# A mixture-of-experts stage whose tiles hold one or two blocks of 128 places

## The chip, the cores and the metric

The kernel runs on one core of a Trainium2 chip. A core has TensorE (PE in the profile; PEld is its weight load), VectorE (DVE), ScalarE (ACT), GpSimd (POOL) and SyncE (SP), which run side by side, keep time by semaphores and share 16 DMA engines. The metric is the device time of one execution in microseconds; less is better.

## The reference

Three computations follow one another: a recurrent attention over 4 x 768 tokens, a mixture of experts with two experts for each token, and a dense network of two layers. The change lies in the second.

```python
def _moe_ref(x, w_gate, w_noise, noise, w1, w2):
    N, D = x.shape            # 3072 tokens, 320 wide; 8 experts, 1024 wide inside
    ...
    top2 = np.argpartition(-noisy_logits, 2, axis=1)[:, :2]
    ...
    for e in range(E):
        for k in range(2):
            mask = top2[:, k] == e
            ...
            h = np.maximum(x[mask] @ w1[e], 0.0)
            out[mask] += top2_w[mask, k, None] * (h @ w2[e])
    return out
```

## The kernel before

The program has three stages, one behind the other. `stage_a` is the attention and leaves each token's row in `xrow` and the gate logits in `LG`. `stage_re` chooses two experts for each token, gives each of the 6144 choices a place in a list ordered by expert, and runs the experts over that list, tile by tile. `stage_m` gathers each token's two results from `ysort`, adds them with their gate weights and runs the dense network.

**Placing.** The list is cut in tiles of `TS` = 256 places, and each expert begins at a new tile. `NTS` = 31 tiles are enough for any choice, and all 31 are always run, whatever the experts' counts are. VectorE counts the choices of each expert (`run`, `cnt`), turns the counts into tiles (`ntile`, `endt`), and from these into each choice's place (`base`, `off`, `pf`, `pos`, L1166 to L1187) and each tile's expert (`ge`, `tef`, `texp`). For the inverse, which token stands in a place, it builds comparisons of the place's low seven bits (`lows`, L1202, four instructions) and of its block of 128 (`highs`, L1194 and L1196 in `columns`, first six blocks and then the rest), and TensorE multiplies them (L1016, 48 matmuls for the six blocks, 48 for the rest). ScalarE copies the first six blocks' tokens to `src` (L1035), VectorE the rest (L1212). GpSimd gathers the tokens' rows to `xs` by them (L1088), SyncE loads the expert's weights by `texp` (L931, L933 the first, L950 the second).

**One tile.** Weights and rows are float32; each is split into a high part of type float32r (ScalarE, `split_hi`, L830) and the rest (VectorE, `split_lo`, L835), and a product takes three matmuls, high by high, high by low and low by high. TensorE runs, for each of `NF` = 8 groups `f` of 128 inner columns, the first layer's eight matmuls (L986 to L990, 256 columns each) into one of four banks; then the six transposes of the next tile's rows (`turn`, L970); then the second layer, for each `f` and each of two blocks `s` three matmuls of 320 columns (L1001 to L1003) into the banks 6 and 7. Beside the first layer ScalarE and VectorE split the second weights (`w2h`, `w2l`) and apply the ReLU and split its result (`hh` L1045, `hl` L1120), in turn for each `f`. Behind the transposes they split the next rows (`xh`, `xl`) and the next first weights (`w1h`, `w1l`), and every second tile a slice of the dense network's weights (`wih`, `woh`, `wil`, `wol`). The split weights have one buffer, so the next first weights are split only after the first layer, and the second weights only after the second; unsplit first weights (`w1t`) and rows (`xs`) have two buffers, unsplit second weights (`w2t`) one, which SyncE loads when VectorE has split the last of the tile before. ScalarE and VectorE carry the result to `ys` (L1058, L1136), and SyncE stores it in `ysort` (L937).

The order of all this is written out by hand. The first two tiles and the last stand alone, the others run in loops (`tiles`), two tiles in each turn, since the buffers alternate. `link` on VectorE makes an instruction wait for the one before.

Of the kernel before, what the change touches and what calls it, by code (L numbers as in the profile page):

```python
# [34 lines left out]
E = 8  # L35
# [6 lines left out]
NTS = (2 * TOK + E * (TS - 1)) // TS  # L42
# [795 lines left out]
def stage_re(nc, st, w_in, w_out, w1, w2, xrow, ysort):  # L838
    ctx = ExitStack()
    with ctx:  # L840
# [11 lines left out]
        NSL, NHI = NT * 128 // TS, NTS * TS // 128  # L852
        NH0 = 6

# [39 lines left out]
        iexp, prev, cnt, ntile, endt, base = (small(E) for _ in range(6))  # L894
        isl, gt = small(NSL), small(E, NSL)
        idx, posl, posh = small(NT, 8).bitcast(U32), small(2, NT).bitcast(U32), small(2, NT).bitcast(U32)
# [6 lines left out]
        ge, tef = small(NTS, E)[0:1], small(NTS)[0:1]  # L903

        ld = [sem("e_ld0"), sem("e_ld1")]
        gx = [sem("e_gx0"), sem("e_gx1")]
        wr = [sem("e_wr0"), sem("e_wr1")]
# [4 lines left out]
        yv = ysort.rearrange("(n s p) m -> n p s m", p=128, s=NS)  # L912
        w2v = w2.rearrange("e (f p) m -> e p f m", p=128)
        LD, GX = 3 * 16, NS * 16

        def tiles(eng, tile):
            tile(0, 0, 0, True, False)
            tile(1, 1, 0, True, False)
            with eng.Fori(1, NTS // 2) as n:
                tile(n * 2, 0, n, False, False)  # L920
                tile(n * 2 + 1, 1, n, False, False)
            tile(NTS - 1, 0, NTS // 2, False, True)

        @block.sync
        def _(sp):
            def tile(i, p, n, first, final):
# [7 lines left out]
                if not first:  # L934
                    sp.wait_ge(q["e_yA"], i - 1)
                    sp.wait_ge(q["e_yV"], i - 1)
                    sp.dma_start(yv[bass.ds(i - 2, 1)].rearrange("o p s m -> (o p) s m"), ys[:, p, :, :]).then_inc(wr[p], 16)  # L937
# [16 lines left out]
            for i in (NTS - 2, NTS - 1):  # L954
                sp.wait_ge(q["e_yA"], i + 1)
                sp.wait_ge(q["e_yV"], i + 1)
                sp.dma_start(yv[i], ys[:, i % 2, :, :]).then_inc(wr[i % 2], 16)
# [4 lines left out]
        def _(pe):  # L962
            mm = nc.tensor.matmul

            def turn(i, p, n):
                pe.wait_ge(gx[p], n * GX + GX)
# [6 lines left out]
            def tile(i, p, n, first, final):  # L973
                if first and p == 0:
                    turn(0, 0, 0)
                pe.wait_ge(q["e_xl"], i * 2 + 2)
                pe.wait_ge(q["e_w1l"], i * 3 + 3)
                for f in range(NF):
                    fs = slice(f * 128, f * 128 + 128)
                    o = ps[2 + f % 4][:, 0:TS]  # L980
# [4 lines left out]
                    for j in range(2):  # L985
                        mm(o, w1h[:, j, fs], xh[:, j, :], start=(j == 0), stop=False)  # L986
                        mm(o, w1h[:, j, fs], xl[:, j, :], start=False, stop=False)  # L987
                        mm(o, w1l[:, j, fs], xh[:, j, :], start=False, stop=False)  # L988
                    mm(o, w1h[:, 2, fs], xh[:, 2, :], start=False, stop=False)
                    mm(o, w1l[:, 2, fs], xh[:, 2, :], start=False, stop=True).then_inc(q["e_mm1"], 1)  # L990
                if not final:
                    turn(i + 1, 1 - p, n + p)
# [28 lines left out]
        def _(act):  # L1021
            def rows_and_w1(i, p, n):
                act.wait_ge(q["e_tr"], i + 1)
                split_hi(nc, xh[:, 0:2, :].rearrange("k j s -> k (j s)"), ps[0][:, :]).then_inc(q["e_xh"], 1)
                split_hi(nc, xh[0:64, 2, :], ps[1][0:64, 0:TS]).then_inc(q["e_xh"], 1)
# [3 lines left out]
            def tile(i, p, n, first, final):  # L1029
# [12 lines left out]
                for f in range(NF):  # L1042
                    split_hi(nc, w2h[:, f, :], w2t[:, f, :]).then_inc(q["e_w2h"], 1)
                    act.wait_ge(q["e_mm1"], i * NF + f + 1)
                    nc.scalar.activation(hh[:, f, :], ps[2 + f % 4][:, 0:TS], ACT.Relu).then_inc(q["e_hh"], 1)  # L1045
                if not final:
                    act.wait_ge(ld[1 - p], (n + p) * LD + LD)
                    rows_and_w1(i + 1, 1 - p, n + p)
# [20 lines left out]
        def _(pool):  # L1069
            iota = nc.gpsimd.iota  # L1070
            iota(iexp, pattern=[[1, E]], base=0, channel_multiplier=0, allow_small_or_imprecise_dtypes=True).then_inc(q["r_io"], 1)
            iota(isl, pattern=[[TS, NSL]], base=0, channel_multiplier=0, allow_small_or_imprecise_dtypes=True).then_inc(q["r_io"], 1)
            iota(itl, pattern=[[1, NHI]], base=0, channel_multiplier=0, allow_small_or_imprecise_dtypes=True).then_inc(q["r_io"], 1)
            iota(i128, pattern=[[1, 128]], base=0, channel_multiplier=0, allow_small_or_imprecise_dtypes=True).then_inc(q["r_io"], 1)
            iota(ids, pattern=[[128, NT]], base=0, channel_multiplier=1, allow_small_or_imprecise_dtypes=True).then_inc(q["r_io"], 1)
            pool.wait_ge(q["r_io"], 5)
# [3 lines left out]
            pool.wait_ge(q["r_src0"], 1)  # L1080
            for i in range(NTS):
                if i == NH0 // NS:
# [3 lines left out]
                for s in range(NS):  # L1086
                    t = NS * i + s
                    pool.indirect_dma_start(out=xs[:, i % 2, s, :], out_offset=None, in_=xrow[:, :],  # L1088
                                            in_offset=bass.IndirectOffsetOnAxis(ap=src[:, t:t + 1], axis=0)).then_inc(gx[i % 2], 16)

        @block.vector
        def _(dve):
# [7 lines left out]
            def rows(i, p):  # L1100
                dve.wait_ge(q["e_xh"], i * 2 + 1)
                split_lo(nc, xl[:, :, :].rearrange("k j s -> k (j s)"), ps[0][:, :],
                         xh[:, 0:2, :].rearrange("k j s -> k (j s)")).then_inc(q["e_xl"], 1)
                dve.wait_ge(q["e_xh"], i * 2 + 2)
                split_lo(nc, xh[64:128, 2, :], ps[1][0:64, 0:TS], xh[0:64, 2, :]).then_inc(q["e_xl"], 1)
# [7 lines left out]
            def tile(i, p, n, first, final):  # L1113
                if first and p == 0:
                    rows(0, 0)
                for f in range(NF):
# [3 lines left out]
                    nc.vector.scalar_tensor_tensor(hl[:, f, :], ps[2 + f % 4][:, 0:TS], 0.0, hh[:, f, :].bitcast(F32),  # L1120
# [386 lines left out]
```

## Time and profile before

| | before |
|---|---|
| three runs | 1484.06 us median (1479.6 to 1484.7) |
| profiled execution | 1484.37 us |
| its span | 1482.5 us, mean granted TensorE clock 0.916 |
| PE busy | 1294.8 us (87%) |
| PEld busy | 1177.1 us (79%) |
| DVE, ACT, POOL busy | 936.5, 656.1, 278.1 us |
| DMA | 197.77 MB, mean 133 GB/s |

The span is the time from the first to the last instruction of the profiled execution; the execution's own time is 1.9 us more. A granted clock of 1.00 is 2.4 GHz and 0.50 is 1.2 GHz. Busy times are means over stages that have different limits, so the table doesn't say what bounds a stage.

### The profile page before, as it was taken

The numbers are of one execution on the slowest core, as the hardware profiler recorded it, in microseconds if no ns is written. First come the engines' busy times: TensorE is split into PE (matmuls) and PEld (weight loads), VectorE is DVE, ScalarE is ACT, GpSimd is POOL, SyncE is SP. The second block draws the span as 40 slices with busy tenths as digits, with TensorE's granted clock in tenths as the row PEclk, the third lists the DMA queues.
The fourth block names the chain that finished last, engine by engine and source line by source line (L and its number), as shares of the span: only waits on it lengthen the run. The fifth ranks groups of instructions, "written<-read, shape, count | busy, mean of one in ns | idle before, by whom it ended". The sixth has DMA issues, their size and how long they took to land. (4 is left out here: it accounts for less than half of the span.)

```text
span 1482.5 us, 40880 instructions
## 1 busy us (share of the span) xinstructions
PE 1294.8 (87%) x16814; PEld 1177.1 (79%) x16814; DVE 936.5 (63%) x1619; ACT 656.1 (44%) x1453; POOL 278.1 (19%) x238
## 2 busy tenths in 40 slices
PE   4468788787989873999999999999949999999998
PEld 3357576666767663999999999999938888888987
DVE  8969485784837007577887878878734444455433
ACT  3334343343543222366776766667613332333332
POOL 1015251432522211211111111111033022020000
PEclk9988787887889975799999999999979999999999
DMA  8572535536242302678777787788612011010000
GB/s 232 137 165 92 144 123 127 171 110 155 87 111 86 113 26 66 186 229 266 229 239 255 222 267 221 248 243 234 218 56 60 19 37 52 3 53 18 0 18 18
DMA packets 158556, 197.77 MB, mean 133 GB/s; under 512 B 62581, under 2 KB 117085, under 8 KB 158429
## 3 DMA queue, kind: packets, MB, share of 16 engines
q1 hardware_dynamic: 133492, 147.96, 33.5%
q10 hardware_dynamic: 19657, 29.90, 6.6%
q0 software_dynamic: 5280, 18.03, 4.3%
q8 instruction: 103, 1.69, 0.5%
q14 instruction: 24, 0.20, 0.0%
HBM read 171.53 MB, written 24.31 MB: 132 GB/s over the span
## 5 line engine op out<-in xcount | busy, mean ns | idle before, releaser
L347 DVE TENSOR_TENSOR prod<-Tl,Lt 128x1 f32<-128x1 f32 (+30 forms) x186 | 143.9, 774 | 59.5 <-DMA Lt<-lscr 53.4
L1295 DVE TENSOR_TENSOR gf<-psM,low 128x512 f32<-128x512 f32 x96 | 66.3, 691 | 181.2 <-ACT low L1333 169.5
L1333 ACT ACTIVATE low<-psM 128x512 f32<-128x512 f32 x96 | 57.5, 599 | 244.4 <-PE psM L1391 223.7
L1001 PE MATMUL psE<-w2h,hh 128*128 128x320 f32 x496 | 155.7, 314 | 0.0
L1003 PE MATMUL psE<-w2h,hl 128*128 128x320 f32 x496 | 153.3, 309 | 0.0
L1002 PE MATMUL psE<-w2l,hh 128*128 128x320 f32 x496 | 153.2, 309 | 0.0
L986 PE MATMUL psE<-xh,w1h 128*128 128x256 f32 x496 | 141.3, 285 | 1.9 <-DVE xh L835 1.9
L987 PE MATMUL psE<-xl,w1h 128*128 128x256 f32 x496 | 141.1, 284 | 0.0
L988 PE MATMUL psE<-xh,w1l 128*128 128x256 f32 x496 | 141.0, 284 | 0.0
L1088 POOL DMA_INDIRECT xs<-xrow,src x62 | 60.9, 983 | 409.5 <-PE psE L970 371.0
L835 DVE TENSOR_TENSOR w2l<-w2t,w2h 128x320 fp32r<-128x320 f32 x248 | 121.9, 492 | 17.5 <-ACT w2h L830 17.5
L1370 PE MATMUL psM<-woh,gh 128*128 128x320 f32 x384 | 120.3, 313 | 4.2 <-DVE gl L835 3.6
L1120 DVE SCALAR_TENSOR_TENSOR hl<-psE,hh 128x256 fp32r<-128x256 f32 x248 | 105.1, 424 | 22.6
L1372 PE MATMUL psM<-woh,gl 128*128 128x320 f32 x384 | 118.7, 309 | 0.0
L1371 PE MATMUL psM<-wol,gh 128*128 128x320 f32 x384 | 118.5, 309 | 0.0
L830 ACT ACTIVATE w2h<-w2t 128x320 fp32r<-128x320 f32 x248 | 114.9, 463 | 6.3 <-DMA w2t<-in_w_dram 5.8
L1045 ACT ACTIVATE hh<-psE 128x256 fp32r<-128x256 f32 x248 | 95.2, 384 | 47.3 <-PE psE L990 46.0
L835 DVE TENSOR_TENSOR w1l<-w1t,w1h 128x1024 fp32r<-128x1024 f32 (+1 forms) x93 | 108.1, 1217 | 2.0
L986 PEld LDWEIGHTS psE<-xh,w1h 128*128 128x128 f32 x496 | 95.9, 193 | 2.3 <-DVE xh L835 2.3
L351 DVE TENSOR_REDUCE Tl<-prod 128x1 f32<-128x1 f32 (+30 forms) x186 | 93.7, 504 | 5.9
L830 ACT ACTIVATE w1h<-w1t 128x1024 fp32r<-128x1024 f32 x93 | 91.4, 1050 | 13.4 <-DMA w1t<-in_w_dram 13.4
L988 PEld LDWEIGHTS psE<-xh,w1l 128*128 128x128 f32 x496 | 95.9, 193 | 0.0
(184 smaller groups left out, 3125.3 us busy)
## 6 DMA issues: line engine op xcount, KB each, us to landing
w2t<-in_w_dram SPq DMA_DIRECT2D x31, 1280.0 KB, 6.8
w1t<-in_w_dram SPq DMA_DIRECT2D x31, 1024.0 KB, 8.7
w1t<-in_w_dram SPq DMA_DIRECT2D x62, 256.0 KB, 9.4
Vd<-in_vG_dram ACTq DMA_DIRECT2D x44, 320.0 KB, 5.3
ysort<-ys SPq DMA_DIRECT2D x31, 320.0 KB, 4.9
RV<-in_rvE_dram ACTq DMA_DIRECT2D x44, 208.0 KB
P<-in_wR_dram SPq DMA_DIRECT2D x24, 209.6 KB
U<-in_wE_dram SPq DMA_DIRECT2D x24, 209.6 KB
```

The costliest lines, as they stand in the source:

```text
L347: mark(nc.vector.tensor_tensor(prod[:, 0:t, 0:t], Tl[:, 0:t, CH - t:CH], Lt[:, t:t + 1, CH - t:CH].to_broadcast([128, t, t]), ALU.mult))
L830: return nc.scalar.activation(hi, src, ACT.Copy)
L835: return nc.vector.tensor_tensor(lo, src, hi.bitcast(F32), ALU.subtract)
L986: mm(o, w1h[:, j, fs], xh[:, j, :], start=(j == 0), stop=False)
L987: mm(o, w1h[:, j, fs], xl[:, j, :], start=False, stop=False)
L988: mm(o, w1l[:, j, fs], xh[:, j, :], start=False, stop=False)
L1001: mm(o, hh[:, f, sl], w2h[:, f, :], start=(f == 0), stop=False)
L1002: mm(o, hh[:, f, sl], w2l[:, f, :], start=False, stop=False)
L1003: m = mm(o, hl[:, f, sl], w2h[:, f, :], start=False, stop=(f == NF - 1))
L1370: mm(o, gh[:, f % 4, sl], woh[:, f, :], start=(f == 0), stop=False)
L1371: mm(o, gh[:, f % 4, sl], wol[:, f, :], start=False, stop=False)
L1372: m = mm(o, gl[:, f % 4, sl], woh[:, f, :], start=False, stop=(f == NF - 1))
```

## The change

A tile may now hold two blocks of 128 places (a pair) or one (a single). An expert's choices begin at a new block, not at a new tile of 256. With blocks of 128, 55 blocks (`NBK`) are enough for any choice; they are run as 23 pairs (`NPR`) and 9 singles (`NSG`), so as 32 tiles. An expert's pairs stand from the front of the list, and where it has an odd block, that one is counted from the end (`send`, `sidx`, `delta`).

The order is fixed in the code (`place`): of every four tiles the second is a single, and in the last four the second and the third. The loops take four tiles a turn. A single runs the same loops with 128 columns in the first layer (`W`), one block in the second, three transposes instead of six, and one gather instead of two; its weights are loaded and split as before. VectorE's copy to `ys` is a memset of one element there.

The table of the tiles' experts now comes from `experts()`, which VectorE runs between the first half and the second half of `lows`; before, its instructions stood in the placement arithmetic.

```diff
-NTS = (2 * TOK + E * (TS - 1)) // TS
+NBK = (2 * TOK + E * 127) // 128
+NSG = 9
+NPR = (NBK - NSG) // 2
+NTS = NPR + NSG
...
-        NSL, NHI = NT * 128 // TS, NTS * TS // 128
+        NSL, NHI = NT, NBK + 1
...
+        def place(u, c, tail):
+            if c == 0 or (c > 1 and not tail):
+                return True, u * 3 + (0, 0, 1, 2)[c]
+            if c == 3:
+                return True, NPR - 1
+            return False, u + c - 1
...
-            with eng.Fori(1, NTS // 2) as n:
-                tile(n * 2, 0, n, False, False)
-                tile(n * 2 + 1, 1, n, False, False)
-            tile(NTS - 1, 0, NTS // 2, False, True)
+            with eng.Fori(1, NU - 1) as u:
+                for c in range(4):
+                    tile(u, c, False, False, False)
+            for c in range(4):
+                tile(NU - 1, c, False, c == 3, True)
...
-                    for s in range(NS):
+                    for s in range(NS if pair else 1):
                         c0 = (j % 2) * TS + s * 128
                         m = nc.tensor.transpose(ps[j // 2][0:kr, c0:c0 + 128], xs[:, p, s, k0:k0 + kr], ident[:, :])
...
+                W = TS if pair else 128
...
-                        mm(o, w1h[:, j, fs], xh[:, j, :], start=(j == 0), stop=False)
...
+                        mm(o, w1h[:, j, fs], xh[:, j, 0:W], start=(j == 0), stop=False)
...
                     pe.wait_ge(q["e_w2l"], i * NF + f + 1)
-                    for s in range(NS):
+                    for s in range(NS if pair else 1):
                         o, sl = ps[6 + s][:, 0:DM], slice(s * 128, s * 128 + 128)
...
-                if i == NH0 // NS:
+                pair, at = place(i // 4, i % 4, i // 4 == NU - 1)
+                if i == 3:
                     pool.wait_ge(q["r_src"], 1)
...
-                nc.vector.tensor_copy(ys[:, p, 1, :], ps[7][:, 0:DM]).then_inc(q["e_yV"], 1)
+                if pair:
+                    nc.vector.tensor_copy(ys[:, p, 1, :], ps[7][:, 0:DM]).then_inc(q["e_yV"], 1)
+                else:
+                    nc.vector.memset(ys[0:1, p, 1, 0:1], 0.0).then_inc(q["e_yV"], 1)
...
+            link(tt(run, pf, thr.rearrange("p (e o) -> p e o", o=1).to_broadcast([128, E, NT]), ALU.is_ge))
+            link(tt(run, run, delta.rearrange("p (e o) -> p e o", o=1).to_broadcast([128, E, NT]), ALU.mult))
+            link(tt(pf, pf, run, ALU.add))
...
+            def experts():
...
+                tt(ge, blk[0:1].rearrange(one_row, o=1).to_broadcast([1, NTS, E]),
+                   pend2[0:1].rearrange("p (o e) -> p o e", o=1).to_broadcast([1, NTS, E]), ALU.is_ge)
...
+                link(ts(tef, tef, float(E - 1), None, ALU.min))
+                nc.vector.tensor_copy(texp[:, :], tef).then_inc(q["r_tx"], 1)
+
             for j in range(2):
+                if j:
+                    experts()
                 for f in (slice(0, 12), slice(12, 24)):
                     tt(lows[:, j, f, :], i128.rearrange("p (o t) -> p o t", o=1).to_broadcast([128, 12, 128]),
...
-        ysort = nc.dram_tensor("ysort", [NTS * TS, DM], F32, kind="Internal").ap()
+        ysort = nc.dram_tensor("ysort", [NBK * 128, DM], F32, kind="Internal").ap()
```

Three places show the new order. The first is VectorE in the placement arithmetic, before, from the table comparison to the position:

```order
L1169 SCALAR_TENSOR_TENSOR w2t<-xs,w2t 128x8
L1170 TENSOR_TENSOR xs<-ys,w2t 1x248
L1172 TENSOR_TENSOR ys<-ys 128x192
L1173 TENSOR_TENSOR w2t<-w2t 128x8
L1174 TENSOR_REDUCE xs<-xs 1x31
L1175 SCALAR_TENSOR_TENSOR w2t<-w2t 128x8
L1176 TENSOR_SCALAR xs<-xs 1x31
L1177 TENSOR_TENSOR ys<-ys,w2t 128x192
L1178 CAST texp<-xs 1x31
L1180 TENSOR_TENSOR ys<-psE,ys 128x192
```

and now (here from the scan of the ends; `w2t`, `xs` and `ys` lend their memory to the small arrays):

```order
L1230 SCALAR_TENSOR_TENSOR w2t<-xs,w2t 128x8
L1231 TENSOR_TENSOR w2t<-w2t 128x8
L1232 TENSOR_TENSOR ys<-ys 128x192
L1233 TENSOR_SCALAR w2t<-w2t 128x8
L1234 TENSOR_TENSOR w2t<-w2t 128x8
L1235 SCALAR_TENSOR_TENSOR w2t<-w2t 128x8
L1236 SCALAR_TENSOR_TENSOR w2t<-w2t 128x8
L1237 TENSOR_TENSOR ys<-ys,w2t 128x192
L1239 TENSOR_TENSOR ys<-psE,ys 128x192
L1240 TENSOR_TENSOR ys<-ys,w2t 128x192
L1241 TENSOR_TENSOR ys<-ys,w2t 128x192
L1242 TENSOR_TENSOR ys<-ys 128x192
```

The rows 1 wide (the tile table) are gone from here, and the three of 192 elements behind `psE` and more rows 8 wide have come.

The second is VectorE at the comparisons: `woh` are the `highs`, `wih` the `lows`. Before:

```order
L1194 TENSOR_TENSOR woh<-ys,w2t 128x48x6
L1196 TENSOR_TENSOR woh<-woh,w2t 128x48x6
L1202 TENSOR_TENSOR wih<-w2t 128x1536 x4
L1194 TENSOR_TENSOR woh<-ys,w2t 128x48x56
L1196 TENSOR_TENSOR woh<-woh,w2t 128x48x56
```

and now, from inside `experts()` on:

```order
L1266 TENSOR_TENSOR xs<-w2t 1x256
L1268 TENSOR_TENSOR xs<-w2t 1x256
L1270 TENSOR_REDUCE xs<-xs 1x32
L1271 TENSOR_REDUCE w2t<-xs 1x32
L1272 TENSOR_TENSOR w2t<-w2t,xs 1x32
L1273 TENSOR_SCALAR w2t<-xs 1x32
L1274 TENSOR_TENSOR w2t<-w2t 1x32
L1275 TENSOR_TENSOR xs<-xs,w2t 1x32
L1276 TENSOR_SCALAR xs<-xs 1x32
L1277 CAST texp<-xs 1x32
L1283 TENSOR_TENSOR wih<-w2t 128x1536 x2
L1256 TENSOR_TENSOR woh<-ys,w2t 128x48x50
```

`texp` is now written between the two halves of the `lows` (the other two `wih` stand ahead of `experts()`), and the second `highs` are 50 blocks wide.

The third is TensorE from the first layer's end to the second layer, before:

```order
L990 MATMUL psE5<-xh,w1l 128x256
L970 MATMUL psE0<-ident,xs 128x128 x4
L970 MATMUL psE1<-ident,xs 64x128 x2
L1001 MATMUL psE6<-w2h,hh 128x320
L1002 MATMUL psE6<-w2l,hh 128x320
L1003 MATMUL psE6<-w2h,hl 128x320
L1001 MATMUL psE7<-w2h,hh 128x320
```

and now, in a single that is followed by a pair:

```order
L1031 MATMUL psE5<-xh,w1l 128x128
L1009 MATMUL psE0<-ident,xs 128x128 x4
L1009 MATMUL psE1<-ident,xs 64x128 x2
L1042 MATMUL psE6<-w2h,hh 128x320
L1043 MATMUL psE6<-w2l,hh 128x320
L1044 MATMUL psE6<-w2h,hl 128x320
L1042 MATMUL psE6<-w2h,hh 128x320
```

The first layer's matmuls have 128 columns, and the second layer stays on bank 6, where it went on to bank 7.

## Rows read from the trace of the kernel before

**Rows 1.** Windows of two stages; columns: span, busy us (count) by engine, PEclk, DMA share, GB/s

```profile
563.00:608.85 45.85, 23.82 (x106) 22.76 (x106) 33.68 (x125) 7.50 (x11) 9.71 (x13) 0.50 0.24 64
608.85:1087.00 478.15, 478.13 (x3652) 477.87 (x3652) 377.91 (x724) 321.99 (x708) 54.61 (x57) 1.00 0.75 235
```

**Rows 2.** Waits in the expert stage: total us, times, longest

```profile
ACT w2h L830 <- DMA w2t<-in_w_dram: 5.8, 2, 4.9
```

**Rows 3.** Timeline of PE, one tile; columns: start, us, engine, line, operation, tiles, count

```profile
1056.75 0.28 PE L986 MATMUL psE<-xh,w1h 128*128 128x256 f32 x1
...
1064.42 0.82 PE L970 MATMUL psE<-ident,xs 128*128 128x128 f32 x6
1065.00 0.39 PE L1001 MATMUL psE<-w2h,hh 128*128 128x320 f32 x1
...
1072.12 0.28 PE L986 MATMUL psE<-xh,w1h 128*128 128x256 f32 x1
```

**Rows 4.** Timeline of DVE in the same tile

```profile
1065.91 0.69 DVE L835 TENSOR_TENSOR xl<-psE,xh 128x512 fp32r<-128x512 f32 x1 [0.45 <-ACT xh L830]
...
1067.12 3.49 DVE L835 TENSOR_TENSOR w1l<-w1t,w1h 128x1024 fp32r<-128x1024 f32 x3
```

**Rows 5.** Windows of L631, of a dense stretch, of the placing matmuls

```profile
194.90:196.90 2.00, 2.00 (x23) 1.91 (x24) 1.71 (x4) 0.55 (x2) 0.00 (x0) 1.00 0.00 0
425.80:473.30 47.50, 43.44 (x1421) 36.61 (x1418) 29.97 (x57) 23.19 (x57) 13.39 (x11) 1.00 0.32 90
584.40:605.40 21.00, 20.57 (x96) 20.51 (x96) 14.69 (x11) 3.13 (x4) 5.04 (x4) 0.50 0.28 68
```

**Rows 6.** Timeline and source view of L631 at full clock

```profile
195.07 1.84 PE L631 MATMUL psA<-wx,xT 104*128 104x96 f32 x15
...
L631 PE MATMUL psA<-wx,xT x16: 275/275/350, 194.9 to 196.6; 104*128 104x96 f32 x16
```

**Rows 7.** Timeline of PE, the placing matmuls

```profile
584.43 10.37 PE L1016 MATMUL psE<-woh,wih 128*128 128x6 f32 x48 [9.26 <-DVE wih L1202]
595.21 10.44 PE L1016 MATMUL psE<-woh,wih 128*128 128x56 f32 x48 [0.40 <-DVE woh L1196]
```

**Rows 8.** Timeline of SP: first weights of tile 0, second weights of a later tile

```profile
579.68 0.43 SPq L931 DMA_DIRECT2D w1t<-in_w_dram  x1
...
1064.96 0.39 SPq L950 DMA_DIRECT2D w2t<-in_w_dram  x1
```

**Rows 9.** DMA issues in the expert stage: count, KB each, median us to landing

```profile
w2t<-in_w_dram SPq DMA_DIRECT2D x29, 1280.0 KB, 6.8
...
w1t<-in_w_dram SPq DMA_DIRECT2D x58, 256.0 KB, 9.4
...
xs<-xrow,src POOLq DMA_INDIRECT x56, 6.4
```

**Rows 10.** Timeline of DVE: placing, and the first tile's split

```profile
577.87 0.14 DVE L1175 SCALAR_TENSOR_TENSOR w2t<-w2t 128x8 f32<-128x8 f32 x1
...
578.61 0.34 DVE L1180 TENSOR_TENSOR ys<-psE,ys 128x192 f32<-128x192 f32 x1
578.98 0.63 DVE L1182 TENSOR_TENSOR w2t<-xs,ys 128x192 f32<-128x192 f32 x2
...
592.20 2.96 DVE L1196 TENSOR_TENSOR woh<-woh,w2t 128x2688 fp32r<-128x2688 f32 x1
...
613.30 0.49 DVE L835 TENSOR_TENSOR w2l<-w2t,w2h 128x320 fp32r<-128x320 f32 x1 [4.48 <-ACT w2h L830]
...
614.04 0.48 DVE L835 TENSOR_TENSOR w2l<-w2t,w2h 128x320 fp32r<-128x320 f32 x1
```

**Rows 11.** Timelines of ACT and POOL before tile 0

```profile
587.22 2.95 ACT L830 ACTIVATE w1h<-w1t 128x1024 fp32r<-128x1024 f32 x3 [13.38 <-DMA w1t<-in_w_dram]
594.84 0.18 ACT L1035 ACTIVATE src<-psE 128x6 uint32<-128x6 f32 x1 [4.68 <-PE psE L1016]
...
596.73 1.02 POOL L1088 DMA_INDIRECT xs<-xrow,src  x1 [0.30 <-issue]
```

More of the change, by code:

```diff
@@ new lines, in slot, with seen @@
+        def slot(u, c, tail=False):
+            pair, at = place(u, c, tail)
+            back = (place(u - 1, c + 2, False) if c < 2 else place(u, c - 2, tail))
+            ahead = place(u, c + 1, tail) if c < 3 else place(u + 1, 0, False)
+            return u * 4 + c, c % 2, u * 2 + c // 2, pair, at, back, ahead
+        def seen(u, c, pair):
+            if not pair:
+                return 16 * (u + 1) if c == 1 else 16
+            return {0: u * 64 + 32, 2: u * 64 + 64, 3: u * 32 + 32}[c]
@@ L924, in _, with store, tile @@
+        def tiles(eng, tile):
+            for c in range(4):
+                tile(0, c, c < 2, False, False)
+            with eng.Fori(1, NU - 1) as u:
+                for c in range(4):
+                    tile(u, c, False, False, False)
+            for c in range(4):
+                tile(NU - 1, c, False, c == 3, True)
         @block.sync
         def _(sp):
-            def tile(i, p, n, first, final):
+            def store(pair, at, p):
+                if pair:
+                    t = yv[at] if isinstance(at, int) else yv[bass.ds(at, 1)].rearrange("o p s m -> (o p) s m")
+                    sp.dma_start(t, ys[:, p, :, :]).then_inc(wr[p], 16)
+                else:
+                    t = yb[2 * NPR + at] if isinstance(at, int) else yb[bass.ds(at + 2 * NPR, 1)].rearrange("o p m -> (o p) m")
+                    sp.dma_start(t, ys[:, p, 0, :]).then_inc(wr[p], 16)
+            def tile(u, c, first, final, tail):
+                i, p, n, pair, at, back, ahead = slot(u, c, tail)
@@ L936, in tile @@
                     sp.wait_ge(q["e_yV"], i - 1)
-                    sp.dma_start(yv[bass.ds(i - 2, 1)].rearrange("o p s m -> (o p) s m"), ys[:, p, :, :]).then_inc(wr[p], 16)
+                    store(*back, p)
                 if p == 0:
@@ L953, in _ @@
             tiles(sp, tile)
-            for i in (NTS - 2, NTS - 1):
+            for c in (2, 3):
+                i, p, n, pair, at, back, ahead = slot(NU - 1, c, True)
                 sp.wait_ge(q["e_yA"], i + 1)
                 sp.wait_ge(q["e_yV"], i + 1)
-                sp.dma_start(yv[i], ys[:, i % 2, :, :]).then_inc(wr[i % 2], 16)
+                store(pair, at, p)
             sp.wait_ge(wr[0], 16 * (NTS - NTS // 2))
@@ L971, in turn, with tile @@
                 m.then_inc(q["e_tr"], 1)
-            def tile(i, p, n, first, final):
+            def tile(u, c, first, final, tail):
+                i, p, n, pair, at, back, ahead = slot(u, c, tail)
+                W = TS if pair else 128
                 if first and p == 0:
-                    turn(0, 0, 0)
+                    turn(0, 0, False)
                 pe.wait_ge(q["e_xl"], i * 2 + 2)
@@ L1085, in _ @@
                     pool.wait_ge(q["e_tr"], i - 1)
[L1086 to L1089, printed above, removed]
+                for z in range(NS if pair else 1):
+                    t = where[2 * at + z if pair else 2 * NPR + at]
+                    pool.indirect_dma_start(out=xs[:, i % 2, z, :], out_offset=None, in_=xrow[:, :],
+                                            in_offset=bass.IndirectOffsetOnAxis(ap=src[:, t:t + 1], axis=0)).then_inc((gx if pair else gs)[i % 2], 16)
         @block.vector
@@ L1111, in first_w, with tile @@
                     split_lo(nc, w1l[0:r, j, :], w1t[0:r, p, j, :], w1h[0:r, j, :]).then_inc(q["e_w1l"], 1)
-            def tile(i, p, n, first, final):
+            def tile(u, c, first, final, tail):
+                i, p, n, pair, at, back, ahead = slot(u, c, tail)
+                W = TS if pair else 128
                 if first and p == 0:
-                    rows(0, 0)
+                    rows(0, TS)
                 for f in range(NF):
```

104 lines of the change are left out of this document (67 added, 37 removed).

## The prediction

> **What bounds the kernel now.** I read the windows by stage first. From 608.85 to 1087.00 us, the expert stage, TensorE is busy for 478.13 of 478.15 us at a granted clock of 1.00; before it lie 45.85 us of gating and placing at clock 0.50 [rows 1]. Then the waits of the expert stage: in no row does TensorE wait; ScalarE waits for it, and for an expert's second weights only twice, 5.8 us together, 4.9 of them in the first tile [rows 2]. So the stage costs what TensorE's stream costs, as long as nothing else comes late.
>
> One tile in the timeline: first layer from 1056.75 to 1064.42, six transposes of the next tile's rows to 1065.00, second layer to 1072.12 [rows 3]. That is 7.67 + 0.58 + 7.12 = 15.37 us a tile, and 31 tiles make 476.5 of the stage's 478.15 (the rest is the first tile at the lower clock).
>
> What waits on the quiet side: ScalarE and VectorE split the next tile's first weights between the transposes and the end of the second layer. VectorE takes the low part of the rows at 1065.91 and ends the last weight difference (L835) at 1067.12 + 3.49 = 1070.61, 1.51 us before TensorE wants it [rows 4]. Counted from the end of the first layer this chain needs 1070.61 - 1064.42 = 6.19 us, with a start-up of TensorE behind it 6.26. The change makes the second layer shorter than that.
>
> **The tiles of one block.** A tile of 128 places still runs 64 matmuls in the first layer, each with 128 columns instead of 256, 24 instead of 48 in the second, and loads and splits the whole of both weights. Every fourth tile is one, and the second to last too.
>
> *First layer.* Each matmul has its own weight load. With 256 columns the pitch is 7.67 / 64 = 0.120 us [rows 3]. No row shows 128 columns of this type at the full clock. The nearest is L631 in the first stage: weights 128 wide, 96 columns, granted clock 1.00 [rows 5]. Fifteen of them in a row, begun at 195.07, take 1.84 us with the last one's 0.275: (1.84 - 0.275) / 14 = 0.112 us [rows 6]. The placing matmuls L1016 say the same at clock 0.50: with 6 columns 48 take 10.37 us, with 56 columns 10.44, about 0.217 each [rows 7], near twice 0.112. Below some width the columns cost nothing and the weight load sets the pitch. So 128 columns should cost 0.112, not half of 0.120. Bounds: 0.067 (half the 256 columns, plus the 0.013 that 0.120 has over 256 columns at 2.4 GHz), and 0.120. I take 0.112, since both rows with few columns sit there: 64 x 0.112 = 7.17 us, a gain of 0.50.
>
> The Trainium skill, "TensorE: Matmul & The Clock Gate", section "Back-to-back issue gap", gives about 81 ns for a pair of weight load and 128-column matmul in a real kernel. By that the first layer would take 64 x 0.081 = 5.2 us, and the whole 9 x 2.0 = 18 us less, 1465. L631's 0.112 speaks against it for 4-byte weights; the same case worked out from rows is the first rival below.
>
> *Second layer.* 24 x 0.146 (7.02 / 48) = 3.51 us instead of 7.02. But the next tile's first layer starts only when its weights are split, 6.26 us after the first layer's end. Behind the three or six transposes (0.58 at most), the second layer ends at 0.66 + 3.51 = 4.17; TensorE then stands idle for 2.1 us. I add 0.07 for the slower first matmul after a gap. So a single tile followed by a pair costs 7.17 + 6.26 + 0.07 = 13.50.
>
> *The second weights.* Their load is issued at 1064.96, 0.54 after the first layer's end, and lands 6.8 us later in the median [rows 8, 9]: 7.34, while the next first layer now starts at 6.26 instead of 7.70. ScalarE's first split of them is then 0.5 us late, but TensorE needs the first low part only for its fifth group, 4 x 0.96 = 3.8 us after its start, that is at 10.1. Nothing is lost, with 2 us to spare.
>
> *Sum.* A pair before a single has three transposes less: 15.37 - 0.29 = 15.08 (8 times). A single before a pair: 13.50 (8 times). The single before a single (tiles 29 and 30) has half the rows to split: 13.50 - 0.29 - 0.27 = 12.94 (0.27 is my estimate for half the row split, of the 1.21 us from 1065.91 to 1067.12 [rows 4], part of which ScalarE's own first split hides). Together 120.64 + 108.00 + 12.94 = 241.6 for 17 tiles, against 16 tiles of before, 245.9; the other pairs stay. **The expert stage gains 4.3 us**, 1% of it, though a tenth of its rows is gone: nine singles save 1.87 each and the thirty-second tile takes nearly all back.
>
> **The placing ahead of it.** All of this runs on VectorE, on the path (TensorE waits 9.26 us for it there [rows 7]).
> - Placement arithmetic: from the block counts to the position, sixteen instructions instead of twelve (the first place of the order). Three 192 wide are new, 3 x 0.37 (578.61 to 578.98, start to start), and so are five 8 wide at 0.09 to 0.18 (L1175 runs 0.14), 0.6; the tile table's four leave, some 0.9, and the comparison of counts is twice as wide, 0.2 with its sum [rows 10]. Net +1.0 us.
> - `experts()`, twelve instructions between the first and second half of the comparisons: four of 256 elements at some 0.37, eight small ones 0.1 to 0.18: +2.7 us.
> - The second `columns` has 50 instead of 56 columns: 2 x 2.96 x 6/56 = -0.6 us [rows 10].
> Together 3.1.
> TensorE's second group of placing matmuls is released by that column work (595.21 [rows 7]), so it starts 3.1 us later and still takes 10.4: **+3.1 us**. The table of experts now comes behind the second quarter of the comparisons and `experts()`: the first quarter released TensorE at 584.43 [rows 7] and will at 585.4; a quarter of 1536 elements takes 1.7 (by 2.96 for 2688 [rows 10]), `experts()` 2.7, so 589.8. Before, the first weights' load followed the table by 1.1 us, was issued at 579.68 and used by ScalarE at 587.22; now 590.9 and 598.4, split by 601.4 [rows 8, 11]. Behind that split in ScalarE's queue stands the copy of the first `src`, which used to run at 594.84, and behind that GpSimd's gathers. The second began 1.9 us after the copy [rows 11], now at 603.3, and by its median of 6.4 us [rows 9] lands at 609.7, against 608.7, when TensorE is through with placing. So this cover is just used up: 0 to 2 us more. I take 3.1, bounds 2 to 5.5.
>
> The end is unchanged: the last tile is a pair, and the gathers behind it read as many rows.
>
> **Result.** -4.3 + 3.1 = -1.2 on the profiled execution's 1484.37 us: 1483.2. The median of the three runs is 1484.06, and they spread over 1479.6 to 1484.7.
>
> **Rivals.**
> 1. *Weight loads don't bind at 128 columns.* Then 0.067 us a matmul, 4.3 us a first layer, but VectorE's two instructions a group (0.73 us from start to start in the first tile, 613.30 to 614.04 [rows 10], about 0.6 with half the columns) hold it to 4.8. That is 2.4 less for each of nine: 22 us, 1461. For it only that the 256-column row can't tell its two causes apart; against it rows 5 and 6.
> 2. *The second weights come late.* With a landing like the first weights' 9.4 us [rows 9] they would arrive at 9.9, the first low part at 11.2, 1.1 after TensorE wants it, and the lag is handed on to the next tile's split. It decides from a landing of about 8.3 us on. Nine times 1.1 to 1.5 is 10 to 13 us, less the 1.2: 1494. For it: 235 GB/s and a DMA share of 0.75 already [rows 1], and the single tiles ask for the same weights in 13.5 instead of 15.4 us. Against it: two late landings in 31 tiles.
> 3. *The clock falls in the single tiles.* At the lower level the first layer's 64 matmuls take 64 x 0.217 = 13.9 us instead of 7.2: nine times 6.7, 1543. For it: during the narrow placing matmuls, TensorE busy 20.57 of 21.00 us, the clock stayed at 0.50 [rows 5]; here too it does narrow work and then idles 2.1 us. Against: in the first stage it held 1.00 over 47.5 us with 4 us idle [rows 5].
> 4. *The pitch stays 0.120*: +4.7 us, 1488. *The start costs 5.5*: 1486. Both remain within no change.
>
> **Chances.** Forecast with its bounds 0.70 (1477 to 1490), first rival 0.08, second 0.12, third 0.03, the rest (something shorter or longer than I see, either way) 0.07. A measurement of this kernel tells about 0.5% (7.4 us) from no change: faster than 1476.6 gets 0.08 and 0.05 from the forecast's edge, slower than 1491.5 gets 0.12, 0.03 and 0.04. Faster 0.13, same 0.68, slower 0.19. The range 1474 to 1494 holds the forecast, the fourth case and most of the second; the first and the third stay out.
>
> **What would show it.** The 128-column matmuls 0.112 apart in the profile after (0.067 to 0.08: first rival). A new idle time of TensorE of about 2 us before the first matmul after each single tile, released by VectorE's last difference at L838 (none: the chain is shorter than I read it). The first matmul of the expert stage at about 612 instead of 608.87. Nearly no wait of ScalarE for the second weights (many: second rival), and clock 1.00 through the stage (else the third). The forecast is wrong if the expert stage isn't within 5 us of 473.8.

## The result, and the profile after

| | before | after |
|---|---|---|
| median of 6 runs | 1479.0 us | 1493.02 us |
| lowest to highest | 1477.74 to 1484.7 | 1489.45 to 1495.16 |
| profiled execution | 1484.37 | 1495.16 |
| its span, granted clock | 1482.5, 0.916 | 1493.2, 0.900 |

The ratio is 1.0078, 95% interval 1.005 to 1.0107: the kernel became slower by 0.8%. The forecast was 1483.2, a little faster than before, with 1474 to 1494 around it. The time is inside the range, but it moved the other way, and the likeliest case, no change, didn't come. Medians and ranges, here and below, are of all executions; the ratios leave out the few that ran in a slower state of the chip, at a lower granted clock.

The two profiled executions differ by 10.8 us. I cut both at the same events. The windows of the kernel after, placing and expert stage (columns as in [rows 1]):

```profile
575.63:614.45 38.82, 23.99 (x107) 22.85 (x107) 28.46 (x59) 4.09 (x7) 4.40 (x5) 0.50 0.27 73
614.45:1100.44 485.99, 469.69 (x3527) 467.11 (x3527) 374.18 (x746) 319.62 (x730) 48.59 (x51) 0.96 0.74 233
```

| part | before | after | difference | forecast |
|---|---|---|---|---|
| up to the count's matmuls, code unchanged | 573.53 | 575.63 | +2.1 | 0 |
| placing, to the first expert matmul | 35.34 | 38.82 | +3.5 | +3.1 |
| expert stage | 478.15 | 485.99 | +7.8 | -4.3 |
| behind it | 395.5 | 392.8 | -2.7 | 0 |

The first and the last part run the same instructions and come out the other way round by about as much; I don't count them as effects. What is to be explained is the expert stage: 12.2 us over its forecast of 473.8. Its clock is 0.96 where [rows 1] has 1.00, and TensorE now stands idle for 16.3 us of it.

The waits in it answer to [rows 2] (total us, times, longest):

```profile
ACT w2h L833 <- DMA w2t<-in_w_dram: 25.8, 11, 4.1
...
PEld psE L1027 <- issue: 18.6, 9, 2.2
...
PE psE L1027 <- DVE w1l L838: 11.8, 6, 2.0
```

A single and what follows it, on TensorE. These rows answer to [rows 3]:

```profile
751.44 0.22 PE L1027 MATMUL psE<-xh,w1h 128*128 128x128 f32 x1
...
758.53 0.84 PE L1009 MATMUL psE<-ident,xs 128*128 128x128 f32 x6
759.13 0.39 PE L1042 MATMUL psE<-w2h,hh 128*128 128x320 f32 x1
...
762.59 0.31 PE L1044 MATMUL psE<-w2h,hl 128*128 128x320 f32 x1
...
764.87 0.38 PE L1027 MATMUL psE<-xh,w1h 128*128 128x256 f32 x1 [1.97 <-DVE w1l L838]
```

The first layer takes 758.53 - 751.44 = 7.09 us, or 0.111 a matmul, the single as a whole 764.87 - 751.44 = 13.43, and TensorE is idle for 1.97 us of it, released by VectorE's last weight difference. All of this is as forecast (7.17, 13.50, about 2). VectorE's chain in the same tile answers to [rows 4]:

```profile
760.04 0.69 DVE L838 TENSOR_TENSOR xl<-psE,xh 128x512 fp32r<-128x512 f32 x1 [0.71 <-ACT xh L833]
...
761.25 3.49 DVE L838 TENSOR_TENSOR w1l<-w1t,w1h 128x1024 fp32r<-128x1024 f32 x3
```

It ends at 764.74, 6.21 us after the first layer's end; it was 6.19 before. What wasn't forecast comes behind the idle time. Windows over it:

```profile
762.90:765.00 2.10, 0.13 (x1) 0.13 (x2) 1.84 (x3) 0.53 (x2) 0.00 (x0) 1.00 1.08 401
765.30:768.50 3.20, 3.20 (x17) 3.20 (x17) 1.34 (x3) 1.27 (x4) 0.00 (x0) 0.50 1.06 369
768.70:774.00 5.30, 5.30 (x46) 5.30 (x45) 4.46 (x11) 4.08 (x12) 0.00 (x0) 1.00 0.34 86
```

TensorE is idle from 762.90, and the clock goes to 0.50 (1.2 GHz) soon after it begins the pair. By the start times sixteen matmuls, from 765.22 to 768.62, are 0.21 apart instead of 0.12; so the clock is back after 3.4 us. The pair's first layer takes 9.27 us instead of 7.77, so the fall costs 1.5. By the start times it happens behind five of the seven singles that stand between pairs in the loop (the pairs at 644.78, 764.87, 825.69, 886.48, 1006.59; those at 705.56 and 947.28 run at full clock): 7.5 us.

The two neighbouring singles at the end lose more (the first is idle for 1.69 us before the second begins):

```profile
1069.00:1075.50 6.50, 6.50 (x33) 6.50 (x32) 3.56 (x11) 2.65 (x11) 0.00 (x0) 0.50 0.51 139
1075.90:1082.50 6.60, 6.60 (x30) 6.53 (x31) 3.27 (x7) 3.37 (x8) 0.00 (x0) 0.50 0.46 142
1082.80:1090.00 7.20, 6.44 (x51) 6.21 (x50) 6.50 (x14) 5.17 (x14) 0.00 (x0) 1.00 0.16 58
```

The clock falls behind the first of them and stays at 0.50 for some 13.6 us, through the whole narrow first layer of the second, though TensorE is busy without a gap. The matmuls are 0.21 apart there:

```profile
1075.05 0.41 PE L1027 MATMUL psE<-xh,w1h 128*128 128x128 f32 x1
1075.26 0.41 PE L1028 MATMUL psE<-xl,w1h 128*128 128x128 f32 x1
```

This tile takes 18.72 us where a single before a pair takes 13.44: 5.3 more. 7.5 + 5.3 = 12.8, and the rest of the forecast was 0.6 too dear: that is the 12.2.

Placing, on TensorE, answers to [rows 7]:

```profile
587.77 5.25 PE L1057 MATMUL psE<-woh,wih 128*128 128x6 f32 x24 [10.49 <-DVE wih L1283]
593.85 5.28 PE L1057 MATMUL psE<-woh,wih 128*128 128x6 f32 x24 [0.83 <-DVE wih L1283]
600.78 10.44 PE L1057 MATMUL psE<-woh,wih 128*128 128x50 f32 x48 [1.65 <-DVE woh L1258]
611.05 1.54 PE L1009 MATMUL psE<-ident,xs 128*128 128x128 f32 x6
```

The wait before the first group is 1.2 us longer (9.26 in [rows 7]): the arithmetic. From the first group to the second it is 13.01 us, where it was 10.78: another 2.2 for `experts()`, less the narrower columns. The transposes of the first rows follow right behind 600.78 + 10.44, so neither the gathers nor the later first weights cost anything.

### The profile page after: what moved, and what is told of

The parts are those of the page before. It is cut to its first block and busy times, and to the rows that moved or that the text cites. A ratio compares the mean times of both kernels' runs of the same rounds, so it can differ in the third digit from the quotient of the medians.

```text
span 1493.2 us, 40450 instructions
## 1 busy us (share of the span) xinstructions
PE 1292.8 (87%) x16689; PEld 1175.6 (79%) x16689; DVE 932.2 (62%) x1657; ACT 653.6 (44%) x1475; POOL 270.2 (18%) x240
## 3 DMA queue, kind: packets, MB, share of 16 engines
q8 instruction: 109, 1.79, 0.5%
## 5 line engine op out<-in xcount | busy, mean ns | idle before, releaser
L1027 PE MATMUL psE<-xh,w1h 128*128 128x256 f32 (+1 forms) x512 | 148.9, 291 | 18.2 <-DVE w1l L838 11.8
L1028 PE MATMUL psE<-xl,w1h 128*128 128x256 f32 (+1 forms) x512 | 148.6, 290 | 0.0
L1029 PE MATMUL psE<-xh,w1l 128*128 128x256 f32 (+1 forms) x512 | 148.5, 290 | 0.0
L1042 PE MATMUL psE<-w2h,hh 128*128 128x320 f32 x440 | 139.2, 316 | 0.0
L1043 PE MATMUL psE<-w2l,hh 128*128 128x320 f32 x440 | 136.5, 310 | 0.0
L1044 PE MATMUL psE<-w2h,hl 128*128 128x320 f32 x440 | 136.4, 310 | 0.0
L1143 POOL DMA_INDIRECT xs<-xrow,src x55 | 53.0, 963 | 427.1 <-PE psE L1009 384.3
L833 ACT ACTIVATE w2h<-w2t 128x320 fp32r<-128x320 f32 x256 | 118.5, 463 | 26.1 <-DMA w2t<-in_w_dram 25.8
L1088 ACT ACTIVATE hh<-psE 128x256 fp32r<-128x256 f32 (+1 forms) x256 | 90.5, 354 | 61.4 <-PE psE L1031 60.8
L1176 DVE SCALAR_TENSOR_TENSOR hl<-psE,hh 128x256 fp32r<-128x256 f32 (+1 forms) x256 | 98.9, 386 | 29.0 <-ACT hh L1088 11.1
L1028 PEld LDWEIGHTS psE<-xl,w1h 128*128 128x128 f32 x512 | 103.1, 201 | 0.0
```

The source lines that it names most:

```text
L833: return nc.scalar.activation(hi, src, ACT.Copy)
L1027: mm(o, w1h[:, j, fs], xh[:, j, 0:W], start=(j == 0), stop=False)
L1028: mm(o, w1h[:, j, fs], xl[:, j, 0:W], start=False, stop=False)
L1029: mm(o, w1l[:, j, fs], xh[:, j, 0:W], start=False, stop=False)
L1042: mm(o, hh[:, f, sl], w2h[:, f, :], start=(f == 0), stop=False)
L1043: mm(o, hh[:, f, sl], w2l[:, f, :], start=False, stop=False)
```

## The experiments

My theory from here on: the gap of 2 us behind a single makes the clock fall. The rivals were late second weights, the narrow matmuls themselves, and something that has to do with the new kernel's order and would not show in the kernel before. A "period" is the time from a tile's first matmul to the next tile's.

**Once more.** The kernel after, unchanged.

> The changed kernel once more, as the measure for the others of this group. Theory: the granted clock of TensorE falls to 0.50 behind some of the singles (in the profile after: the first layer of the next tile takes 9.2 to 9.3 instead of 7.8 us behind five of the eight, and one longer stretch behind the two singles in a row), some 12 us in all. Where these stretches lie should differ from execution to execution, their sum not much: 1490 to 1495 us, 5 to 8 of the tiles behind a single slow. Rival (the slow tiles have a fixed cause, such as late weights): the same tiles slow as in the profile after.

Measured: 1495.51 us (1491.01 to 1500.23, 8 runs), ratio 1.0092 (1.0053 to 1.0131). The stage:

```profile
612.24:1098.20 485.96, 469.72 (x3527) 467.13 (x3527) 374.67 (x746) 319.51 (x730) 48.54 (x51) 0.96 0.73 233
```

Again five of the seven pairs are slow, but not the same five (the tiles at 642.60, 762.70, 823.50, 943.60 and 1004.40: the sixth single's is in, the fifth's out), and the neighbour takes 18.67. So the fall isn't tied to one tile; how often it comes is nearly fixed, where is not. The table-early run at the end of this section, with the same idle time of 1.97 us, has four of the seven slow.

**The gap filled.** TensorE does work that nobody reads, behind the second layer of a single; bank 7 isn't used there.

```diff
+                for _ in range(0 if pair else 3):
+                    mm(ps[7][:, 0:384], ident[:, :], LG[:, :, :].rearrange("p i e -> p (i e)"), start=True, stop=True)
```

> Behind the second layer of each single TensorE runs three more matmuls of plain float32 (identity by 384 columns of the old logits, into the unused bank 7), about 1.95 us, so that it does not stand idle; nothing reads the result. Theory (the idle 2 us bring the clock down): the period of a single stays 13.4 to 13.5, the clock is 1.00 through the whole expert stage, and the time is 12 us less than the changed kernel's, about 1481. Rival (the narrow first layer of 128 columns brings it down): the clock still falls and the time stays at 1493.

Measured: 1481.27 us (1474.28 to 1487.63), ratio 0.9992 (0.9954 to 1.003); in the same group of runs the kernel after took 1495.51.

```profile
609.91:1083.34 473.43, 473.04 (x3581) 462.81 (x3581) 373.16 (x746) 319.20 (x730) 48.64 (x51) 1.00 0.76 239
```
```profile
756.60 0.31 PE L1044 MATMUL psE<-w2h,hl 128*128 128x320 f32 x1
756.75 2.10 PE L1047 MATMUL psE<-LG,ident 128*128 128x384 f32 x6
758.88 0.38 PE L1027 MATMUL psE<-xh,w1h 128*128 128x256 f32 x1
```

The second matmul row is the filling, 2.10 us long (the three float32 matmuls have two records each); the next tile begins when it would have begun anyway. No tile is slow, the clock is 1.00, and the stage is 12.6 us shorter: 473.43 against a forecast of 473.8. This is the experiment that settles the cause. VectorE's chain, the weight loads and the tiles are as without it, and ScalarE waits as often for the second weights (12 times, 26.1 us; 11 times, 25.8 us without it); only the idle time is gone. So late second weights aren't the cause. It also shows that the rest of the stage's sum was right.

**A third of the filling** (one matmul instead of three, 0.65 us, so that some 1.3 us stay idle). One execution.

> As the filled gap, but one extra matmul of 384 columns instead of three (some 0.65 us), so that about 1.35 of the 2.0 us of idle time stay (0.65 of that work stands in their place). Theory: the shorter the idle time, the fewer the falls of the clock: none or one or two of the eight tiles behind a single slow (9.2 us), against five in the profile after, and an expert stage of 474 to 478 us. Rival (any idle time brings it down): five or more slow.

```profile
614.88:1092.95 478.07, 467.68 (x3545) 462.07 (x3545) 372.75 (x746) 318.91 (x730) 48.55 (x51) 0.98 0.75 237
```

The whole execution took 1491.41 us against 1484.01 for one of the kernel before, too few to compare. None of the seven pairs is slow; the second of the neighbouring singles still is (18.46). So 2 us of idleness bring the fall about most of the time and 1.3 us, in front of a pair, didn't once in seven. Before the second of the neighbours 1.0 us was idle, and there the clock fell.

**The singles' first layer at 256 columns,** everything else as after.

```diff
-                    o = ps[2 + f % 4][:, 0:W]
+                    o = ps[2 + f % 4][:, 0:TS]
...
-                        mm(o, w1h[:, j, fs], xh[:, j, 0:W], start=(j == 0), stop=False)
+                        mm(o, w1h[:, j, fs], xh[:, j, :], start=(j == 0), stop=False)
```

> The singles' first layer runs with 256 columns, of which the last 128 are left over from an earlier tile and are not used; the idle time of 2 us stays. Theory (idle time): clock falls as before, and each single's first layer takes 7.68 instead of 7.10 us: 9 x 0.58 = +5 us, 1498. Rival (narrow matmuls): the clock stays at 1.00, 1493 + 5 - 12 = 1486.

Measured: 1495.21 us (1491.14 to 1507.16), ratio 1.0076 (1.004 to 1.0111).

```profile
614.14:1104.41 490.27, 472.63 (x3527) 470.12 (x3527) 375.68 (x746) 320.21 (x730) 48.66 (x51) 0.97 0.73 231
```

A single now takes 14.00 instead of 13.44, so the narrow first layer was worth 0.56. The idle time stays at 2.0 us and all seven pairs fall, and the last tile too; so narrow matmuls ahead of the gap aren't what makes the clock fall. The second of the neighbours stayed at full clock this time, with 1.69 us idle before it; that is why the time stayed under the 1498 that I expected. So this run doesn't show whether a wide one would have recovered sooner.

**The kernel before with gaps.** In every second tile the second layer runs one block; the other block's result is left out.

```diff
-                    for s in range(NS):
+                    for s in range(NS if p == 0 else 1):
```

> The kernel before, with one change: in every second tile (15 of 31) the second layer runs one block only, so the other block's result is left out. All matmuls keep their width, the placing is the old one. Theory: each such tile has an idle time of 2.0 us and a period of 7.67 + 6.26 + 0.07 = 14.0 instead of 15.37 us, 15 x 1.37 = 20.6 us less, but behind five or more of eight of them the clock falls for 3.4 us and the next first layer takes 9.25: 15 x 0.6 to 0.9 x 1.5 = 14 to 20 us back, so 1472 to 1481. Rival (the fall needs the narrow matmuls or the new layout): the clock stays, 1481.6 - 20.6 = 1461.

Measured: 1478.61 us (1469.92 to 1487.63) against 1477.97, ratio 1.0014 (0.9988 to 1.004).

```profile
599.60:1075.80 476.20, 446.55 (x3292) 442.44 (x3292) 377.08 (x724) 319.58 (x708) 54.53 (x57) 0.95 0.75 236
```
```profile
753.20:756.40 3.20, 3.20 (x17) 3.20 (x17) 1.35 (x4) 1.21 (x3) 0.00 (x0) 0.52 1.04 387
757.00:762.00 5.00, 5.00 (x44) 5.00 (x43) 4.26 (x11) 3.72 (x11) 0.00 (x0) 1.00 0.39 113
```

The short tiles take 13.99 us, 1.97 idle, and 12 of 15 are followed by the same slow stretch. Fifteen tiles save 15.37 - 13.99 each, 20.7 us; twelve falls give 12 x 1.5 = 18 back; the stage is 2.0 us shorter than in [rows 1]. Nothing of the change is in this kernel but the gap. TensorE is busy for 31.6 us less than in [rows 1], and the kernel is no faster.

**All tiles full.** The order and places of after, but each single computes two blocks.

> The changed kernel, with TensorE doing the work of a full tile in the singles too (256 columns, two blocks, six transposes; the second block is left over from an earlier tile and not used). Placing, gathers, order and tile count are the new ones. Theory: no idle time, clock 1.00 through the stage, 32 x 15.37 us plus the first tile's 1.6: 493.5 us for the expert stage, and the placing's 3.5 us: 1481.6 + 15.4 + 3.5 = 1500. Then 15.4 and 3.5 are what the one tile more and the placing cost. Rival (something else of the new order slows tiles): periods over 15.37.

Measured: 1495.52 us (1489.8 to 1504.23), ratio 1.0133 (1.0088 to 1.0178).

```profile
601.84:1095.21 493.37, 493.37 (x3770) 493.10 (x3770) 378.23 (x746) 321.08 (x730) 48.68 (x51) 1.00 0.73 229
```

Every period is 15.37 and the clock 1.00. The thirty-second tile, the loops of four and the load order cost exactly one tile; singles as they are bring only 7.4 of 493.4 us.

**First weights in halves.** With the two halves of the columns split one after the other, TensorE may start on the first.

```diff
-                pe.wait_ge(q["e_w1l"], i * 3 + 3)
+                pe.wait_ge(q["e_w1l"], i * 6 + 3)
...
+                    if f == NF // 2:
+                        pe.wait_ge(q["e_w1l"], i * 6 + 6)
...
-                for j in range(3):
-                    split_hi(nc, w1h[:, j, :], w1t[:, p, j, :]).then_inc(q["e_w1h"], 1)
+                for h in (slice(0, F1 // 2), slice(F1 // 2, F1)):
+                    for j in range(3):
+                        split_hi(nc, w1h[:, j, h], w1t[:, p, j, h]).then_inc(q["e_w1h"], 1)
```

> The first weights are split in two halves of their columns, and TensorE starts the first layer when the first half is there and waits for the second before its fifth group. Theory: the chain behind a single's first layer shortens from 6.2 to about 4.3 us, the idle 2.0 us go to 0 to 0.5, and with them the falls of the clock: 9 x 1.5 to 1.9 plus 12 us, 1493 - 27 = 1466, faster than the kernel before (1479). Rival (narrow matmuls bring the clock down): only 14 to 17 us are won, 1477.

Measured: 1471.65 us (1461.65 to 1487.35), ratio 0.9919 (0.9876 to 0.9961). Its profiled execution is the slowest of these (1487.35), and it reaches the expert stage some 10 us later than the kernel after did, so I read only that stage:

```profile
624.70:1090.14 465.44, 461.42 (x3527) 458.63 (x3527) 373.92 (x839) 324.31 (x823) 50.34 (x51) 0.98 0.77 243
```

A single before a pair takes 11.80 with 0.33 idle. Of the pairs only the first is clearly slow, and not by the clock, which stays at 1.00: TensorE stands still for 0.83 us within its first layer. In the second of the neighbours the clock still falls. There ScalarE waits for the second weights, and TensorE, through `hl`, for ScalarE and VectorE:

```profile
1061.32 0.47 ACT L833 ACTIVATE w2h<-w2t 128x320 fp32r<-128x320 f32 x1 [2.37 <-DMA w2t<-in_w_dram]
```
```profile
1062.66 0.30 PE L1029 MATMUL psE<-xh,w1h 128*128 128x128 f32 x1 [0.75 <-DVE hl L1181]
```

Behind this stall the clock is at 0.50 for 10.24 us. Here the late second weights of my second rival reach TensorE, and a stall of 0.75 us inside a narrow first layer is followed by a fall, where 0.83 us inside the wide one was not.

**Halves, and the singles apart:** the tail runs pair, single, pair, single.

```diff
-            if c == 0 or (c > 1 and not tail):
+            if c == 0 or c == 2 or (c == 3 and not tail):
                 return True, u * 3 + (0, 0, 1, 2)[c]
-            if c == 3:
-                return True, NPR - 1
-            return False, u + c - 1
+            return False, u + (c == 3)
```

> The first weights in halves, as before in this study, and the last four tiles in the order pair, single, pair, single, so that no single follows a single and the last one has nothing behind it. Theory: the stretch at clock 0.50 in the second of the two neighbours (period 17.0) goes, and the last single costs 7.1 + 3.8 us with no idle time: 42.9 us for the last three tiles become 38.3, 4.6 less than with halves alone: 1467. Rival (that stretch had another cause than the neighbours' stall): no change against 1471.65.

Measured: 1466.23 us (1461.04 to 1472.99), ratio 0.9912 (0.9885 to 0.9939). It computes the whole result, and it beats both kernels.

```profile
613.28:1073.29 460.01, 456.33 (x3527) 453.15 (x3527) 374.56 (x839) 323.84 (x823) 49.91 (x51) 1.00 0.78 246
```
```profile
758.10 0.38 PE L1027 MATMUL psE<-xh,w1h 128*128 128x256 f32 x1 [0.34 <-DVE w1l L838]
```

The stage is 26.0 us shorter than after. Against the filled gap it is 13.4: nine times the 1.6 us by which a single is shorter would be 14.4. The other half of the 26 is the clock. The late second weights show once more: behind the first single they hold TensorE up for 0.73 us in the middle of a wide first layer. Behind five of the others the first layer is 0.1 to 0.35 longer; behind the second single, with 0.34, ScalarE had again waited for its second weights, for 2.31 us. The clock stays at 1.00.

**Halves in the kernel before,** the same edit.

> The kernel before with its first weights split in halves. Theory: its tiles have no idle time, the periods stay 15.37 us and the time is that of before within 0.3% (three more small instructions a tile on each of ScalarE and VectorE lie beside TensorE). Rival (the gain of the halves has nothing to do with the singles): up to 1% faster.

Measured: 1480.04 us, ratio 0.9997 (0.997 to 1.0024); all periods 15.37. There VectorE ended 1.5 us ahead of need, so an earlier start is worth nothing. The halves and the singles only gain together.

**The table early.** `texp` is a constant, `experts()` is left out, so all tiles run expert 0's weights. One execution.

> The changed kernel with a constant table of experts (all tiles run expert 0), written at the start of the placing, and without experts(), so its 2.7 us and the later load of the first weights are both gone. Theory: from the first count matmul to the first matmul of the experts 38.8 us become 36.5 (the placement arithmetic's 1.2 stay, the 2.2 of experts() less the shorter columns go). Rival (the late weights or gathers count): less than 36, down to the 35.3 of before.

```profile
568.42 1.01 PE L1049 MATMUL psE<-ys,xs 128*128 128x192 f32 x2 [13.72 <-DVE ys L1219]
...
580.58 20.64 PE L1057 MATMUL psE<-woh,wih 128*128 128x6 f32 x96 [10.51 <-DVE wih L1282]
601.05 1.54 PE L1009 MATMUL psE<-ident,xs 128*128 128x128 f32 x6
```

The expert stage begins at 604.45, 36.03 us behind the start of the count's matmuls instead of 38.82. So `experts()` is 2.8 of the 3.5 us of placing. The other 0.7 are the arithmetic (10.51 us of waiting against 9.26 in [rows 7], 1.25) less some 0.55 for the narrower columns. 36.03 lies between my 36.5 and the rival's "less than 36"; the whole, 1489.12 us, is one execution. In its expert stage four of the seven pairs are slow, and the second of the neighbours takes 19.88.

## Why the prediction was wrong

The step that failed is the idle time behind a single. The sum entered it with its length alone and put what it does to the granted clock at nothing; the runs show 12.2 to 12.8 us for that term. By the sign that I had set, an expert stage within 5 us of 473.8, the forecast is wrong at 485.99. That 1493.02 us lies inside 1474 to 1494 is luck: the upper end was drawn for late second weights, which cost nothing here.

**Right: the width of the first layer.** 0.111 us a matmul where I took 0.112, and not 0.067. The first rival is out. The Trainium skill, "TensorE: Matmul & The Clock Gate", section "Back-to-back issue gap", has about 81 ns for a pair of weight load and 128-column matmul; the rows of this case disagree, with 0.111 us at full clock.

**Right: the chain that sets a single's length.** 6.21 us to VectorE's last difference, periods of 13.43, 15.04 and 12.82 where 13.50, 15.08 and 12.94 were forecast. With the gap filled the stage takes 473.43 us against 473.8. The thirty-second tile takes back what the singles save, as I had it.

**Right: placing.** +3.5 against +3.1, by the terms named (arithmetic 1.25 against 1.0, `experts()` 2.8 against 2.7, columns -0.55 against -0.6), and the cover for gathers and first weights held.

**Second rival: half right, and harmless.** ScalarE's waits for second weights went from 2 to 11 times. But the median landing is 6.9 us, under the 8.3 from which it would decide, and filling the gap alone brought the stage to its forecast though ScalarE waited 12 times. Only in the two versions with halves, where the tiles are shorter still, do these waits reach TensorE, by 0.1 to 0.83 us a time.

**Wrong: the third rival, "the clock falls in the single tiles".** I gave it 0.03. It is what happened, and three things in my treatment failed.

First, the argument against it. I wrote that the first stage "held 1.00 over 47.5 us with 4 us idle" [rows 5]. The row is right, but the mean hides what decides. 1.6 of these 4 us stand in its last 3.4 us, as one piece, and the clock falls just where my window ends:

```profile
425.80:469.90 44.10, 41.63 (x1346) 35.15 (x1343) 26.71 (x53) 22.59 (x56) 13.38 (x11) 1.00 0.34 96
469.90:473.30 3.40, 1.81 (x75) 1.46 (x75) 3.26 (x5) 0.60 (x1) 0.01 (x1) 1.00 0.05 15
473.30:476.50 3.20, 3.20 (x24) 2.49 (x25) 3.10 (x4) 0.50 (x2) 0.00 (x0) 0.52 0.00 0
```
```profile
471.41 0.71 PE L648 MATMUL psA<-TT,Xs 128*40 128x128 f32 x9 [1.61 <-issue]
```

So the row that I took as evidence against the rival ends with a case for it. Four more windows of the attention stage:

```profile
217.60:220.70 3.10, 2.24 (x31) 1.96 (x35) 3.00 (x5) 1.10 (x5) 2.52 (x2) 1.00 0.00 0
220.90:224.00 3.10, 2.30 (x99) 1.50 (x90) 3.07 (x3) 0.84 (x1) 2.18 (x1) 0.50 0.75 194
528.20:531.30 3.10, 1.76 (x127) 1.32 (x118) 0.00 (x0) 0.00 (x0) 2.06 (x1) 1.00 0.02 5
531.60:538.00 6.40, 6.22 (x73) 4.87 (x76) 0.00 (x0) 1.80 (x4) 0.73 (x1) 0.50 0.01 3
```

TensorE was idle for 0.9 us of the first and 1.3 us of the third stretch, and both are followed by 0.50. It isn't so every time: TensorE had also been idle for 1.79 us in one piece before a matmul at 143.39, and there the clock stayed up.

```profile
140.60:143.70 3.10, 1.31 (x15) 0.94 (x16) 2.98 (x4) 2.35 (x5) 0.57 (x1) 1.00 0.37 133
143.70:149.90 6.20, 6.11 (x139) 5.20 (x133) 5.96 (x8) 2.60 (x7) 0.00 (x0) 1.00 0.03 7
```

With these rows a new gap of 2 us in every fourth tile could not have had 0.03.

Second, the price. I took the low clock for all of a single's first layer, nine times, 60 us. It falls behind the single, in the next tile, lasts 3.4 us and costs 1.5 when that tile is a pair, and 5.3 when it is narrow. The whole is 12.8. A mechanism with a wrong price of 60 us looks absurd beside the other cases; with the right one it is the rival that turns a gain of 1 us into a loss of 11.

Third, I asked for each gap what the idle time costs (2 us, entered in the sum) but not what it does to the engine's speed behind it, though I had seen in [rows 5] that this chip has a low level and can stay on it.

**Not settled.** Why four or five of seven fall and the others don't, with the same 1.97 us idle and the same instructions ahead. And what the fall in the second neighbour rests on: with 1.0 us of idle time it came, before pairs with 1.3 us it didn't. That it stays low so long there goes with its narrow matmuls, but each run has only this one place for it, so the width as the reason isn't shown. The unchanged stretches before and behind differ by +2.1 and -2.7 us between the two profiled executions; I didn't look for a reason.

## What to carry to other kernels

An idle time that the change adds to TensorE in the middle of a dense stream can have two prices: its length, and a slow start of what follows. Look in the trace at hand for the falls of the granted clock and at the few microseconds ahead of each, never at a mean over tens of microseconds. When work is taken from the engine that bounds a stage, work out which chain comes next (here VectorE's weight split); shortening that one first, or filling the gap, decides whether the change pays: after 1.0078, gap filled 0.9992, chain shortened 0.9919, and with the two neighbouring singles also set apart 0.9912.

## What the runs showed of the hardware

A gap of 1.97 to 2.04 us between float32r matmuls at full clock was followed by a fall to 0.50 in 5 of 7 (after), 5 of 7 (once more), 4 of 7 (table early), 8 of 8 (singles at 256 columns, the last pair with them) and 12 of 15 places (the kernel before with gaps). With 256-column matmuls behind it, the clock came back after about 3.4 us. With 128-column matmuls behind a gap of 1.69 us, 0.21 apart and without a further gap, it did not come back during the first layer of 11.7 us; it did in the 320-column second layer. That is one place in each run. It fell in none of 7 places with 1.33 us idle before a pair, never where the gap was filled, and not in the version with halves and singles apart, where the gap was 0.34 us.

128 columns of float32r take 0.111 us with a weight load each, 256 columns 0.120, at full clock. At half clock the pitch is 0.21 to 0.22, whatever the width from 6 (the placing matmuls) to 256 columns (the first layer of the slow pairs).
